# A fused RWKV, soft-MoE and FFN kernel: bonus values of the first chunk on ScalarE, and the bonus vector spread by a matmul

## What is computed

```python
state = zeros((B, H, D, D))
for t in range(S):
    kt, vt, rt = k[:, :, t], v[:, :, t], r[:, :, t]
    cur = einsum('bhd,bhe->bhde', u[None] * kt, vt)
    y[:, :, t] = einsum('bhd,bhde->bhe', rt, state + cur)
    state = w[None, :, :, None] * state + einsum('bhd,bhe->bhde', kt, vt)
```

## Time and profile before

| | us |
|---|---|
| three runs | 385.68, 383.95, 385.41 |
| median | 385.41 |
| profiled execution | 385.27 |
| its span | 383.5 |

### The profile page before, as it was taken

The page is one execution under the profiler, slowest core; times in us unless marked ns, Lnnn a source line. Parts: engine busy times, 40 slices in busy tenths (PEclk is TensorE's granted clock), DMA queues, the critical chain, the costliest instruction groups (busy, mean ns, idle before and its releaser), DMA issues.

```text
span 383.5 us, 9099 instructions
## 1 busy us (share of the span) xinstructions
PE 369.9 (96%) x3206; PEld 290.6 (76%) x3206; DVE 235.0 (61%) x433; ACT 189.4 (49%) x409; POOL 94.5 (25%) x110
## 2 busy tenths in 40 slices
PE   5698999999999999999999999999999999999996
PEld 5677788878777344577888888888888888888885
DVE  6978787878774301587756556555555555555550
ACT  1344554545434440676564456445644564465452
POOL 4678788878682020100000000000000000000000
PEclk9999999999999999999999999999999999999999
DMA  7899999999999999600011002000200020002002
GB/s 234 286 333 344 400 393 405 399 393 354 405 327 409 390 414 413 249 0 2 1 46 38 0 0 84 0 0 0 82 0 0 0 82 0 0 0 82 0 2 82
DMA packets 21797, 63.76 MB, mean 166 GB/s; under 512 B 3088, under 2 KB 6816, under 8 KB 21392
## 3 DMA queue, kind: packets, MB, share of 16 engines
q1 hardware_dynamic: 20864, 63.09, 43.4%
q10 hardware_dynamic: 912, 0.39, 0.5%
HBM read 58.75 MB, written 4.72 MB: 165 GB/s over the span
## 4 chain that ended last, share of the span: by engine, by line
PE 92%; DVE 2%; DMA 2%; issue 1%; ACT 1%; POOL 1%; SPq 0%; DVEq 0%; ACTq 0%
PE bank L638 11%; PE bank L637 11%; PE bank L636 11%; PE bank L378 6%; PE pair L426 6%; PE pair L636 6%; PE pair L637 6%; PE pair L638 6%; PE bank L623 4%; PE pair L414 3%; PE pair L397 3%; PE bank L585 3%; PE bank L447 3%; PE bank L565 2%; DMA vb<-v 2%; PE bank L438 2%
## 5 line engine op out<-in xcount | busy, mean ns | idle before, releaser
L926 DVE TENSOR_TENSOR gf<-bank,sg 128x512 f32<-128x512 f32 x72 | 49.8, 691 | 58.3 <-ACT sg L1133 58.0
L1133 ACT ACTIVATE sg<-bank 128x512 f32<-128x512 f32 x72 | 42.9, 598 | 71.0 <-PE bank L623 71.0
L637 PE MATMUL bank<-ghi,whi 128*128 128x512 f32 x190 | 73.9, 389 | 0.0
L636 PE MATMUL bank<-glo,whi 128*128 128x512 f32 x190 | 73.9, 389 | 0.0
L638 PE MATMUL bank<-ghi,wlo 128*128 128x512 f32 x190 | 73.9, 389 | 0.0
L937 DVE TENSOR_TENSOR glo<-gf,ghi 128x512 fp32r<-128x512 f32 x96 | 66.3, 691 | 0.3
L1139 ACT ACTIVATE ghi<-gf 128x512 fp32r<-128x512 f32 x95 | 59.3, 624 | 1.8 <-DVE gf L926 1.7
L636 PEld LDWEIGHTS bank<-glo,whi 128*128 128x128 f32 x190 | 35.7, 188 | 7.4
L637 PEld LDWEIGHTS bank<-ghi,whi 128*128 128x128 f32 x190 | 35.7, 188 | 7.4
L638 PEld LDWEIGHTS bank<-ghi,wlo 128*128 128x128 f32 x190 | 35.7, 188 | 7.4
L772 DVE TENSOR_TENSOR rks<-rkb,bank 112x512 f32<-112x512 f32 x48 | 30.8, 681 | 15.4 <-PE pair L414 10.9
(11 more groups left out here) (179 smaller groups left out, 512.3 us busy)
## 6 DMA issues: line engine op xcount, KB each, us to landing
ring<-w SPq DMA_DIRECT2D x24, 512.0 KB, 6.3
rkb<-rk SPq DMA_DIRECT2D x23, 512.0 KB, 6.2
krb<-kr SPq DMA_DIRECT2D x24, 384.0 KB, 5.5
ring<-w SPq DMA_DIRECT2D x4, 1536.0 KB, 14.3
ring<-w SPq DMA_DIRECT2D x8, 768.0 KB, 8.4
vb<-v SPq DMA_DIRECT2D x24, 192.0 KB, 5.5
out<-ob SPq DMA_DIRECT2D x18, 256.0 KB, 2.1
ring<-win SPq DMA_DIRECT2D x3, 1024.0 KB, 14.3
```

The source lines that it names most:

```text
L636: pe.matmul(o, w_hi, lo, start=(f == 0), stop=False)
L637: pe.matmul(o, w_hi, hi, start=False, stop=False)
L926: dve.tensor_tensor(gf[:, f % 2, :], bank[f % 4][:, :], sg[:, f % 2, :], ALU.mult).then_inc(gf_ok, 1)
L1133: act.activation(sg[:, f % 2, :], bank[f % 4][:, :], ACT.Sigmoid, scale=1.702).then_inc(sg_ok, 1)
```

## The change

- u is loaded on one partition only (1.5 KB). VectorE clears `ubc` and fills `et` with ones ahead of its other memsets; PE multiplies the ones by `ubc`, which puts u on all partitions in PSUM, and ScalarE copies it back into `ubc`. PE warms up with 5 matmuls ahead of that product and one behind it, and with 6 in place of 7 after the first transposes.
- In all steps GpSimd multiplies by `ubc`; VectorE no longer does so in the first chunk.
- In the first chunk GpSimd no longer makes `vd`. ScalarE does, by eight activations of 128x48 with the bonus number as scale, at the end of its own step, behind `columns` and `rows`.
- VectorE's order in the first chunk: scaling of the next step, then the masks, then this step's bonus sum (in step (0,0) the sum ahead of the masks); before, the next step's sum stood at the end.
- The state isn't decayed for steps (0,0) to (0,2), when it is zero.
- SyncE's order in the first chunk: `rkb` of steps (0,2), (0,3) and (1,0) go ahead of the `krb` of the step before them; in the loop `rkb` of the following step ends a step, where it began the next one.

```diff
-WARM = 10
+WARM = 5
             def step(c, b, first, count):
-                load_rk(c, b)
+
                 load_kr(c, b)
                 load_v(c, b)
                 load_w1(first, count)
+                if not (is_last(c) and b == B - 1):
+                    load_rk(*following(c, b))
...
-            step(0, 2, 0, 0)
-            step(0, 3, 0, 0)
+            load_rk(0, 2)
+            load_v(0, 2)
+            load_rk(0, 3)
+            load_kr(0, 2)
+            load_v(0, 3)
+            load_rk(1, 0)
+            load_kr(0, 3)
...
             keep_warm(LG, WARM)
+
+            pe.wait_ge(ones_ok, 1)
+            pe.wait_ge(s_u, 16)
+            pe.matmul(YN[:, 0:DM], et[:, :], ubc[:, :, :].rearrange("p h e -> p (h e)"), start=True, stop=True)\
+              .then_inc(u_ps, 1)
+            keep_warm(LG, 1)
...
                     pe.wait_ge(wks_done, 1)
+                    pe.wait_ge(u_ok, 1)
...
-                    keep_warm(LG, 7)
+                    keep_warm(LG, 6)
...
-                wait(pe, vd_ok, n + 1)
+                wait(pe, *((vd_first, n + 1) if is_first(c) else (vd_ok, n - B + 1)))
...
+            dve.memset(ubc[:, :, :], 0.0).then_inc(u_clear, 1)
+            dve.memset(et[:, :], 1.0).then_inc(ones_ok, 1)
...
             def bonus_sum(c, b):
                 n = B * c + b
-                if is_first(c):
-
-                    dve.wait_ge(rk_ok, n + 1)
-                    if b == 0:
-                        dve.wait_ge(s_const, 16 * 2)
-                    dve.tensor_tensor(rkn[:, b % 2, :, :], rkn[:, b % 2, :, :], ubc[:, :, :], ALU.mult)\
-                       .then_inc(rku_ok, 1)
                 dve.wait_ge(rku_ok, n + 1)
-                wait(dve, vd_ok, n - 1)
+                wait(dve, vd_used, n - 1)
                 dve.tensor_reduce(dds[:, b % 2, :], rkn[:, b % 2, :, :], AX_X, ALU.add).then_inc(dd_ok, 1)
...
-                dve.wait_ge(sdec, HP * (n + 1))
+
+                if is_first(c):
+                    dve.wait_ge(s_new, 1)
+                else:
+                    dve.wait_ge(sdec, HP * (n - B + 2))
...
-                if is_first(c) and b:
+                if is_first(c):
+
+                    scale(*following(c, b))
+                    if b == 0:
+                        bonus_sum(c, b)
                     mask(c, b)
-                    scale(*following(c, b))
+                    if b:
+                        bonus_sum(c, b)
...
-                if more:
+                if more and tail:
                     bonus_sum(*following(c, b))
...
+                if is_first(c) and b == B - 1:
+                    bonus_sum(*following(c, b))
...
             scale(0, 0)
...
-            bonus_sum(0, 0)
...
-            for dst, src in ((ubc[:, :, :].rearrange("p h e -> p (h e)"), u.partition_broadcast(P)),
-                             (keep[:, :], strict)):
-                act.dma_start(dst, src).then_inc(s_const, 16)
+            act.dma_start(keep[:, :], strict).then_inc(s_const, 16)
+            act.wait_ge(u_clear, 1)
+            act.dma_start(ubc[0:1, :, :].rearrange("p h e -> p (h e)"), u.partition_broadcast(1)).then_inc(s_u, 16)
+            act.wait_ge(u_ps, 1)
+            act.activation(ubc[:, :, :].rearrange("p h e -> p (h e)"), YN[:, 0:DM], ACT.Copy).then_inc(u_ok, 1)
...
+            def bonus_values(c, b):
+
+                n = B * c + b
+                act.wait_ge(dd_ok, n + 1)
+                act.wait_ge(v_in[b], 16)
+                wait(act, vd_used, n - 1)
+                if b == 0:
+                    act.wait_ge(zeroed, 5)
+                for w in range(2):
+                    for x in range(HP):
+                        h = HP * w + x
+                        last = act.activation(vd[:, b % 2, x, w, 0:D], vb[:, b, h, :], ACT.Copy,
+                                              scale=dds[:, b % 2, h:h + 1])
+                last.then_inc(vd_first, 1)
...
-                    if not is_last(prev(c, b)[0]):
+                    if not is_first(prev(c, b)[0]) and not is_last(prev(c, b)[0]):
                         decay(*prev(c, b))
                     columns(*prev(c, b))
...
                         rows(*prev(*prev(c, b)))
+                if not tail:
+                    bonus_values(c, b)
...
-                if is_first(c):
-                    return
                 pool.wait_ge(rk_ok, n + 1)
+                if is_first(c, b):
+                    pool.wait_ge(u_ok, 1)
                 pool.tensor_tensor(rkn[:, s, :, :], rkn[:, s, :, :], ubc[:, :, :], ALU.mult).then_inc(rku_ok, 1)
...
-                bonus_values(c, b)
+                if not is_first(c):
+                    bonus_values(c, b)
```

More of the change, by code:

```diff
@@ L192, in rwkv_soft_moe_ffn @@
             sem(n) for n in ("lt_ps", "l_ok", "cm_ok", "nm_ok", "ex_ok", "al_ok", "tr_ps", "tr_ok", "p_ps", "run_ok"))
+        u_clear, ones_ok, s_u, u_ps, u_ok = (sem(n) for n in ("u_clear", "ones_ok", "s_u", "u_ps", "u_ok"))
+        vd_first = sem("vd_first")
         nm_new, l_new, mask_go, tiles_go = (sem(n) for n in ("nm_new", "l_new", "mask_go", "tiles_go"))
@@ L791, in mask @@
                     dve.wait_ge(zeroed, 5)
-                    dve.wait_ge(s_const, 16 * 2)
+                    dve.wait_ge(s_const, 16)
                 for half in range(2):
@@ L1223, in bonus_values @@
                 wait(pool, vd_used, n - 1)
-                if is_first(c, b):
-                    pool.wait_ge(zeroed, 5)
                 pool.tensor_tensor(vd[:, b % 2, :, :, 0:D].rearrange("p x w e -> p w x e"),
```

## The result

| | before | changed |
|---|---|---|
| median of 7 runs, us | 385.68 | 389.22 |
| lowest to highest | 383.95 to 386.38 | 387.88 to 391.81 |
| profiled execution | 385.27 | 389.39 |
| its span | 383.5 | 387.6 |
| mean granted clock of TensorE | 1.000 | 0.986 |

The ratio is 1.0109, with a 95% interval of 1.0085 to 1.0134: the change makes the kernel 1.1% slower. The forecast was 385.8 us, no change, in a range that ended at 388.2.

The account below looks back on a forecast made before the run. TensorE was taken to bound the kernel from scores (1,1) on. Start-up and first-chunk terms moved these from 33.40 to 33.85 us, +0.4: 385.7 against the profiled 385.27, 385.8 for the median; range 382.8 to 388.2.

Parts of the forecast that it names:

- What bounds the kernel: TensorE's endless queue of work from scores (1,1) on; whatever moves its start moves the end by the same amount.
- the landmark: Scores of step (1,1), at 33.40 us before, where TensorE gets its endless queue of work; expected at 33.85.
- The start-up: 0 to 12 us: `rkb` scaled at 5.2 instead of 6.77 us, ScalarE at its first bonus values at 10.9.
- rival B: Start-up: `rkb` lands as before, ScalarE's chain comes 1.4 us later, scores (1,1) at 35.25, 387.2 us; chance 0.17.
- ScalarE's pieces: First chunk: eight bonus-value activations of 128x48 per step take 1.93 us, bounds 1.8 and 2.6.
- The chain of the first chunk: 12 to 33 us: it becomes ScalarE's, and L397 of step (0,3) ends at 28.1 instead of 26.1 us.
- The step that failed: End of first chunk: L414 to scores (1,1) takes 5.75 us of TensorE's own work without the stall, giving 33.85.
- Rival E: Start-up: TensorE's scores and transposes of (0,0) run at the slow pace, 1.2 us more, 387.0 us; chance 0.08.
- Rival C: Around the loop's first pass: TensorE's instructions arrive late, the stall ends at 35.0 to 35.6, 387.5 us; chance 0.13.
- Rival D: First chunk: ScalarE's pieces overlap more or its queue doesn't wait as assumed; 2.2 us faster, 383.2 us; chance 0.12.

Follow-up runs that it names:

- e2: The changed kernel with GpSimd instead of ScalarE making the first chunk's bonus values; 384.41 us, ratio 0.9987.
- e1: The changed kernel with 24 unused matmuls in TensorE's four first-chunk waits for ScalarE's vd; 385.77 us, ratio 1.0020.
- e11: e10 with eleven unused matmuls filling TensorE's idle stretch; 386.40 us, ratio 1.0032.
- e10: The kernel before, with TensorE's second L397 of step (0,3) held by eighteen small unused ScalarE activations; 389.06 us, ratio 1.0079.
- e9: The changed kernel with, in the first chunk, VectorE's sums ahead of masks and ScalarE's bonus values ahead of columns and rows; 384.32 us, ratio 0.9974.
- e4: The kernel before with only the start-up changed: u loaded on one partition and spread by matmul, five warm-up matmuls; 384.58 us, ratio 0.9977.
- e14: e9 with seven unused matmuls in TensorE's wait of step (0,1) and nine in that of step (0,3); 383.71 us, ratio 0.9965.
- e15: e4 with 4, 7 and 3 unused matmuls ahead of scores (0,1), (0,2) and (0,3); 383.64 us, ratio 0.9973.
- e5: The kernel before, with TensorE's second L397 of step (0,3) held by ten small unused ScalarE activations; 386.37 us, ratio 1.0046.
- e13: The changed kernel with nine unused matmuls in only the last and longest of TensorE's four waits for vd; 386.23 us, ratio 1.0027.
- e3: The changed kernel with ScalarE's rows of the first chunk behind its bonus values instead of ahead; 387.96 us, ratio 1.0073.

## Why the prediction was wrong

**What bounds the kernel.** Right for this change: the end moved by what the landmark moved, 4.1 us for 4.13. Behind it the distance to before stays: 4.19 us at a scores group of 88.66 us before (92.85 after), and 4.06 at the first of the experts' matmuls (132.19 against 128.13). For a landmark that comes earlier it holds less well (e2).

**The start-up.** Right on `rkb` (5.2 expected, 5.23 measured), so rival B fell. Short on TensorE: I took 0.20 us for a warm-up record from a mean of twenty, of which the last ran at the fast pace. The ten took 2.50 us, not 2.0, and the spreading matmul 1.62, not 1.2. Scores (0,0) began at 7.30 instead of 6.65, and ScalarE's first bonus values at 11.64 instead of 10.9.

**ScalarE's pieces.** Right: 1.91 us for eight, expected 1.93. The estimate from the Trainium skill's page "VectorE: DVE Perf Modes" (section "The TRN2 errata"), 1.8, was 0.1 us short.

**The chain of the first chunk.** Right in kind and nearly in size. The four L397 (now L413) were expected to start at 12.95, 17.3, 22.4 and 27.5 us, and started at 13.61, 18.35, 23.34 and 28.33. The 0.66 us lost in the start-up runs through all of them. To it comes 0.5 us in the first step, which the sum did not have: behind the wait of 1.92 us the clock fell, and from L413 to the columns are 2.21 us (13.61 to 15.82) in place of the 1.71 taken from the kernel before. The three steps behind it were each about 0.1 us shorter than reckoned. That leaves the 0.83 us of the fourth.

**The step that failed** is the next one: from that L414 (26.10) to scores (1,1) without the stall is 5.75 us of PE's own work. The 5.75 was read from a stretch with the clock at 1.00 and moved behind a wait that the same sum had just made more than 2 us long. With the 0.6 us of L397 ahead of it the sum had 6.35 us. At the full clock it was 6.25 (e1 and e11), and as the change leaves it 9.20. The 2.85 us from 6.35 to 9.20, with the 0.83 by which the fourth L413 was late, are the 3.68 us between 33.85 and 37.53. What the sum had at nothing is the price of the slow clock.

**Rival E** had the mechanism and the wrong place and price. I looked for the clock only in the start-up, where the warm-up was halved, at 1.2 us. In the profiled execution of the changed kernel the part from scores (0,0) to `wkn` took 1.94 us (7.30 to 9.24) in place of 1.73, so 0.2 us of it came true. It can come in full: in the profiled execution of e2 it took 3.06 us (7.56 to 10.62), and in that of e10, whose warm-up is the old one, 3.05 (8.34 to 11.39). So halving the warm-up need not be its cause. It didn't occur to me that a chain on ScalarE means idle stretches on TensorE several times over.

**Rival C**, the slower side, fell: there is no stall in the changed kernel. The instruction packet on which it built moves at 30 to 31 us, before the stall begins at 31.85 and not just ahead of its end. What it said of the place holds in part: e9 shows the stall 12 records later, where the program ahead of it is 16 records shorter and has a few waits more. The Trainium skill ("Runtime: NRT & Kernel Launch", section "Instruction fetch mechanics") has instructions fetched in blocks of 256, and a stall that moves with the program would fit that. In e2, whose order of work on TensorE is that of e9, the same group of scores takes 1.65 us in place of 1.16, which fits too. What makes the stall come or go stays open. It isn't only that TensorE comes late: in e4, e14 and e15 TensorE starts scores (1,1) at 30.17 to 30.96 us, earlier than in e9, and no such stall shows.

**Rival D** fell: ScalarE's queue does wait as written. An order that removes most of these waits (e9) brings the time down from 389.2 to 384.3.

**Gains that came.** u's load alone brings the kernel to 0.9977. That the product off VectorE and the new orders add to this isn't shown: with the bonus values on GpSimd the changed kernel is at 0.9987, and its interval (0.9970 to 1.0004) takes in no gain at all. Whatever the parts gained, the change as a whole lost it through one part.

## What to carry to other kernels

When a sum makes the busiest engine wait longer, the work behind the wait must be priced at the clock that it will have there, not at the one of the trace before. Look at which engine's idle stretches a moved piece creates: work that fits into a free engine can still leave TensorE standing. A handful of matmuls without use in such a wait tells within one run whether the clock is the loss, and may be worth keeping where the wait can't be removed. Not every fall of the clock is worth it, though: between e4 and e15, where TensorE waits for VectorE in the first chunk, filling the waits changed nothing.

## What the runs showed of the hardware

- TensorE's granted clock fell to 0.50 (1.2 in place of 2.4 GHz) behind idle stretches of 2.47 us in the changed kernel and 2.37 us in e10, and stayed there for the next 6.6 us (28.30 to 34.90) and 6.4 us (29.05 to 35.50). Behind shorter idle stretches it fell in some executions and not in others. It held behind 1.38 us in the changed kernel, 1.64 us in e5 and 1.75 us in the kernel before, and it fell behind 1.38 us in e13, 1.69 us in e3 and 1.74 us in e4.
- The price was 2.95 us on 6.25 us of work at the full clock. That is less than twice the time, since the clock came back within it.
- In the start-up matmuls can run at the slow pace while the profile gives a clock of 1.00: in e10 the first scores took 2.08 us in place of 1.16.
- The load of one 1536-byte row to 128 partitions, 192 KB, held up a load of 512 KB beside it: without it VectorE could use `rkb` at 5.20 us (e4) in place of 6.77. In some executions it still came a little later, at 5.58 us in e9.
- A stall of TensorE's instruction stream of 0.5 to 1.2 us stood near the first pass of a loop in the kernel before and in e9, 12 records apart. In the changed kernel, e4, e14 and e15 it did not show; what decides it is open.
